# Routing moved into the last dense expert, with a scratch region for every routed expert

## What is computed

```python
x = attention(r, k, v, w, u)                  # [1536 tokens, 384]
P = sinkhorn(exp(x @ w_gate))                 # dense mixture: every token, every expert
x = sum(P[:, e:e+1] * (relu(x @ w1[e]) @ w2[e]) for e in range(8))
xn = x / (norm(x) + 1e-6)                     # routed mixture
logits = xn @ en.T / tau                      # en: 8 unit vectors
idx = argmax(logits, axis=1)
gate = softmax(logits)[token, idx]
out[token] = gate * (relu(x @ w1b[idx]) @ w2b[idx])
```

## Time and profile before

| | us |
|---|---|
| median of 3 runs | 1227.06 (1222.53 to 1227.62) |
| the profiled execution | 1222.38 |
| its span, first to last instruction | 1220.6 |
| PE busy | 1152.3 (94%) |
| DVE busy | 506.7 (42%) |
| ACT busy | 424.8 (35%) |
| POOL busy | 228.2 (19%) |

### The profile page before, as it was taken

One profiled execution on the slowest core, in us unless ns is written; L12 is line 12 of the kernel. 1 busy time (PEld: TensorE's weight loads), 2 busy tenths in 40 slices (PEclk: granted clock), 3 DMA queues, 4 the chain that ended last, 5 costly groups with the idle time before them and its releaser, 6 DMA issues. The chain is left out here.

```text
span 1220.6 us, 18206 instructions
## 1 busy us (share of the span) xinstructions
PE 1152.3 (94%) x6862; PEld 1024.9 (84%) x6862; DVE 506.7 (42%) x881; ACT 424.8 (35%) x860; POOL 228.2 (19%) x229
## 2 busy tenths in 40 slices
PE   6998899999999999999999999999999953999997
PEld 5887769899999998999999899999999822899997
DVE  6777555221222222222212222222222253999996
ACT  4655342212212211211221221222111133988884
POOL 4555252102202201210220220121000013010001
PEclk9889899999999999999999999999999975999999
DMA  9620060200020030020002002000000017999991
GB/s 227 124 59 15 2 204 25 102 2 1 1 104 1 1 104 2 1 104 1 1 16 88 2 1 104 1 1 1 1 1 1 1 65 288 368 374 361 368 354 63
DMA packets 97285, 107.91 MB, mean 88 GB/s; under 512 B 53033, under 2 KB 85710, under 8 KB 97216
## 3 DMA queue, kind: packets, MB, share of 16 engines
q1 hardware_dynamic: 95232, 102.15, 25.3%
q0 software_dynamic: 1984, 4.75, 1.0%
HBM read 98.37 MB, written 9.89 MB: 89 GB/s over the span
## 5 line engine op out<-in xcount | busy, mean ns | idle before, releaser
L809 DVE SCALAR_TENSOR_TENSOR h_lo<-hid,h_hi 128x512 fp32r<-128x512 f32 x192 | 132.8, 691 | 571.9 <-ACT h_hi L745 571.9
L745 ACT ACTIVATE h_hi<-hid 128x512 fp32r<-128x512 f32 x192 | 115.0, 599 | 633.9 <-PE hid L859 633.9
L872 PE MATMUL acc<-w_hi,h_hi 128*128 128x384 f32 x768 | 260.4, 339 | 0.0
L872 PE MATMUL acc<-w_hi,h_lo 128*128 128x384 f32 x768 | 260.1, 339 | 0.0
L872 PE MATMUL acc<-w_lo,h_hi 128*128 128x384 f32 x768 | 259.4, 338 | 0.0
L859 PE MATMUL hid<-x_hi,w_lo 128*128 128x512 f32 x576 | 227.6, 395 | 0.0
L859 PE MATMUL hid<-x_lo,w_hi 128*128 128x512 f32 x576 | 227.3, 395 | 0.0
L859 PE MATMUL hid<-x_hi,w_hi 128*128 128x512 f32 x576 | 226.7, 394 | 0.4 <-issue 0.4
L721 POOL TENSOR_TENSOR w_lo<-raw,w_hi 128x384 fp32r<-128x384 f32 x112 | 114.8, 1026 | 556.1 <-ACT w_hi L737 556.1
L872 PEld LDWEIGHTS acc<-w_lo,h_hi 128*128 128x128 f32 x768 | 144.1, 188 | 8.9
L872 PEld LDWEIGHTS acc<-w_hi,h_hi 128*128 128x128 f32 x768 | 144.1, 188 | 8.1
(11 more groups left out here) (214 smaller groups left out, 1282.1 us busy)
## 6 DMA issues: line engine op xcount, KB each, us to landing
raw<-in_moe_w SPq DMA_DIRECT2D x54, 1536.0 KB, 8.9
rows<-filler SPq DMA_DIRECT2D x19, 194.0 KB, 9.1
m_x<-rows SPq DMA_DIRECT2D x19, 194.0 KB, 5.0
spread_w<-in_w SPq DMA_DIRECT2D x16, 144.0 KB, 3.2
spread_r<-in_r SPq DMA_DIRECT2D x16, 144.0 KB, 2.9
spread_k<-in_k SPq DMA_DIRECT2D x16, 144.0 KB, 3.0
v_sb<-in_v SPq DMA_DIRECT2D x16, 144.0 KB, 3.4
out_y<-m_y,m_token POOLq DMA_INDIRECT x19, 6.9
```

The source lines that it names most:

```text
L745: act.activation(h_hi[st % HB][:, :], hid[st % HB][:, :], ACT.Relu).then_inc(s_hhi, 1)
L809: dve.scalar_tensor_tensor(h_lo[st % HB][:, :], hid[st % HB][:, :], 0.0, h_hi[st % HB][:, :].bitcast(F32), ALU.max, ALU.subtract).then_inc ...
L872: mm = pe.matmul(acc[j][:, 0:DM], a[st % HB][:, j * P:(j + 1) * P], b[q][1][:, f * DM:(f + 1) * DM], start=(f == 0 and x == 0), stop=(f == ...
```

## The change

`route` is gone and its work is spread over the last dense expert (`last_expert` on ACT, DVE and PE).

- **Units.** The 12 tiles form six units (`UNITS`): tiles 0 to 3, tiles 4 to 7, and tiles 8, 9, 10 and 11 by themselves. For each unit run `square` and `roots` on ACT, `turn_tile` on PE, `columns` on ACT, `score` on PE (tiles as the stationary operand, so that logits come out by token), `scales` and `choose` on DVE, `exps` on ACT, `rank` on PE, `weigh` and `locate` on DVE, and one indirect DMA for each tile. Logits are no longer scaled before the maximum; 1/tau is in the expert vectors and the norm in the exponential's scale.
- **Place.** Unit 0 is worked off in steps 9 to 15, unit 1 in steps 17 to 23 and right after. The last group's `hidden` steps run one after the other without `outward` between them, with five more h_hi and h_lo buffers in the space of `x_hi` and `x_lo`; then each of the last four tiles gets its 24 `outward` matmuls in one piece, with the routing of the tile before in between. `keep_clock` puts matmuls whose result nobody reads between the last small ones.
- **Ranks.** A running count `seen` is multiplied in on PE, so a token's row is known when its tile is, because each expert now has a region of 1536 rows in `rows`. The block counts are needed only for slots 8 to 18: slots 0 to 7 are the first block of each expert, in order.
- **Scratch.** `rows` has 12416 rows in place of 2432, filled by one DMA of 2.4 MB for each expert.
- **Weights.** Experts 0 and 1 of the routed mixture are loaded during the last dense expert, and expert 0 is split there by ACT and POOL. In the routed stage slot `s` takes its raw weights from the other buffer, and the splitting of slot 0 is gone.
- **Hand-over.** The wait for the scatters is now SP's, in the routed stage. PE starts that stage with 8 matmuls of 256 fp32 columns (`WARM`) ahead of `turn_x(0)`.

```diff
+        def fill(sp, e):
+            one = slice(e * REGION, (e + 1) * REGION) if isinstance(e, int) else bass.ds(e * REGION, REGION)
+            sp.dma_start(rows[one, :].rearrange("(t p) c -> p t c", p=P),
+                         filler[:, :].unsqueeze(1).broadcast_to([P, REGION // P, ROW])).then_inc(s_fill, 16)
...
-            for n in range(SLOTS):
-                sp.dma_start(rows[n * P:(n + 1) * P, :], filler[:, :]).then_inc(s_fill, 16)
-            sp.wait_ge(s_fill, 16 * SLOTS)
+            sp.dma_start(tau_col[:, :], tau.unsqueeze(0).broadcast_to([E, 1])).then_inc(s_tau, 16)
+            sp.dma_start(rows[E * REGION:E * REGION + P, :], filler[:, :]).then_inc(s_fill, 16)
+            for n in range(2):
+                fill(sp, n)
             with sp.Fori(2, E) as e:
                 sp.wait_ge(s_wlo, (e - 1) * NP)
                 load_expert(sp, w1, w2, e, raw, s_raw)
+                fill(sp, e)
+            sp.wait_ge(s_wlo, LAST * NP)
+            load_expert(sp, w1_next, w2_next, 0, raw, s_raw)
+            sp.wait_ge(s_wlo, E * NP)
+            load_expert(sp, w1_next, w2_next, 1, raw, s_raw2[0])
...
                 split(i * 2 + 2, 0)
             split(E - 1, 1)
+            split(E, 0)
+            pool.wait_ge(s_fill, 16 * (E + 1))
+            for u, (a, b) in enumerate(UNITS):
+                pool.wait_ge(s_gate, u + 1)
+                pool.wait_ge(s_pos, u + 1)
+                for t in range(a, b):
+                    pool.indirect_dma_start(
+                        out=rows, out_offset=bass.IndirectOffsetOnAxis(ap=pos_i[:, t:t + 1], axis=0),
+                        in_=out[:, t, :], in_offset=None).then_inc(s_scat, 16)
...
+            def square(t):
+                act.wait_ge(s_out, LAST * AC + t + 1)
+                if t:
+                    act.wait_ge(s_ssq, t)
+                act.activation(t_sq[:, :], out[:, t, 0:DM], ACT.Square, accum_out=ssq[:, t:t + 1]).then_inc(s_ssq, 1)
+            def roots(u):
+                a, b = UNITS[u]
+                act.wait_ge(s_ssq, b)
+                act.activation(root[:, a:b], ssq[:, a:b], ACT.Sqrt).then_inc(s_root, 1)
+            def columns(t):
+                act.wait_ge(s_tr, t + 1)
+                act.activation(x_cols[t % 2][:, :], bank_of(t)[:, XT:XT + DM], ACT.Copy).then_inc(s_xt, 1)
+            def exps(u):
+                act.wait_ge(s_sh, u + 1)
+                for t in range(*UNITS[u]):
+                    ex = act.activation(expd[:, t, :], shifted[:, t, :], ACT.Exp, scale=scale[:, t:t + 1],
+                                        accum_out=esum[:, t:t + 1])
+                ex.then_inc(s_exp2, 1)
...
+            def last_expert(e, q):
...
+                for t in range(2 * GT, TT):
+                    u = unit_of(t)
+                    square(t)
+                    roots(u)
+                    columns(t)
+                    exps(u)
...
+            def scales(u):
+                a, b = UNITS[u]
+                dve.wait_ge(s_root, u + 1)
+                done[0] = newton(dve, s_rstep, done[0], root[:, a:b], ssq[:, a:b], guess[:, a:b], quot[:, a:b])
+                rstep(dve.reciprocal(scale[:, a:b], quot[:, a:b]))
+            def choose(u):
...
+                dve.wait_ge(s_lg, b)
+                rstep(dve.tensor_reduce(top[:, a:b], lg, AX.X, ALU.max))
+                dve.tensor_tensor(shifted[:, a:b, :], lg, top[:, a:b].unsqueeze(2).broadcast_to([P, n, E]), ALU.subtract).then_inc(s_sh, 1)
+                dve.wait_ge(s_sh, u + 1)
+                flat = hit[:, a:b, :].rearrange("p t e -> p (t e)")
+                rstep(dve.tensor_scalar(flat, shifted[:, a:b, :].rearrange("p t e -> p (t e)"), 0.0, None, ALU.is_ge))
+                rstep(dve.tensor_tensor_scan(order[:, 0:n * E], again[:, 0:n * E], flat, 0.0, ALU.mult, ALU.add))
+                dve.scalar_tensor_tensor(flat, order[:, 0:n * E], 1.0, flat, ALU.is_equal, ALU.mult).then_inc(s_hit, 1)
+            def weigh(u):
+                a, b = UNITS[u]
+                dve.wait_ge(s_exp2, u + 1)
+                rstep(dve.tensor_scalar(esum[:, a:b], esum[:, a:b], 1e-9, None, ALU.add))
+                dve.reciprocal(out[:, a:b, DM], esum[:, a:b]).then_inc(s_gate, 1)
+            def locate(u):
...
+            def last_expert(e):
...
+                        locate(0)
+                scales(1)
+                choose(1)
+                weigh(1)
+                locate(1)
+                tail_add(2 * GT)
+                for t in range(2 * GT, TT):
+                    u = unit_of(t)
+                    scales(u)
+                    choose(u)
+                    if t + 1 < TT:
+                        tail_add(t + 1)
+                    weigh(u)
+                    locate(u)
...
-            with dve.Fori(1, E) as e:
...
+            def turn_tile(t):
+                pe.wait_ge(s_out, LAST * AC + t + 1)
...
+                for k in range(KD):
+                    mm = pe.transpose(bank_of(t)[:, XT + k * P:XT + (k + 1) * P], out[:, t, k * P:(k + 1) * P], ident[:, :])
+                mm.then_inc(s_tr, 1)
+            def score(t):
...
+                pe.wait_ge(s_xt, t + 1)
+                for k in range(KD):
+                    mm = pe.matmul(bank_of(t)[:, at:at + E], x_cols[t % 2][:, k * P:(k + 1) * P], e_cols[:, k, :],
+                                   start=(k == 0), stop=(k == KD - 1), skip_group_check=True)
+                mm.then_inc(s_lg, 1)
+            def rank(u):
...
+                bank = bank_of(a)
+                pe.wait_ge(s_hit, u + 1)
+                if u:
+                    pe.wait_ge(s_seen, u)
+                tokens = lambda c: hit[:, a:a + c, :].rearrange("p t e -> p (t e)")
+                mm = pe.matmul(bank[:, RK:RK + n * E], upper[:, :], tokens(n), start=True, stop=False, skip_group_check=True)
+                for d in range(1, n):
+                    mm = pe.matmul(bank[:, RK + d * E:RK + n * E], ones[:, :], tokens(n - d), start=False, stop=False,
+                                   skip_group_check=True)
+                for d in range(n):
+                    mm = pe.matmul(bank[:, RK + d * E:RK + (d + 1) * E], ones[:, :], seen[u][:, :], start=False, stop=True,
+                                   skip_group_check=True)
+                mm.then_inc(s_rank, 1)
+            def last_expert(e, q):
...
+                for st in range(TAIL, FL - 1):
+                    hidden(e, q, st + 1)
+                    if TAIL + 2 <= st < TAIL + 2 + GT:
+                        score(st - TAIL - 2 + GT)
+                    if TAIL + 1 <= st < TAIL + 1 + GT:
+                        turn_tile(st - TAIL - 1 + GT)
+                for j in range(GT):
+                    t = TAIL // KF * GT + j
+                    pe.wait_ge(s_out, e * AC + (NG - 2) * GT + j + 1)
+                    for f in range(KF):
+                        st = TAIL + f
+                        if j == 0:
+                            pe.wait_ge(s_hlo, e * FL + st + 1)
+                        for x, (a, b) in enumerate(((h_hi, hi), (h_hi, lo), (h_lo, hi))):
+                            h = h_buf(a, x_hi if a is h_hi else x_lo, st)
+                            mm = pe.matmul(acc[j][:, 0:DM], h[:, j * P:(j + 1) * P], b[q][1][:, f * DM:(f + 1) * DM],
+                                           start=(f == 0 and x == 0), stop=(f == KF - 1 and x == 2))
+                        if f == KF - 1:
+                            mm.then_inc(s_tacc, 1)
+                        if f == 1:
+                            if j == 0:
+                                rank(1)
+                            if j >= 2:
+                                rank(unit_of(t - 2))
+                            if j >= 1:
+                                turn_tile(t - 1)
+                        if f == 5 and j >= 1:
+                            score(t - 1)
+                keep_clock(2)
+                rank(unit_of(TT - 2))
+                turn_tile(TT - 1)
+                keep_clock(2)
+                score(TT - 1)
+                keep_clock(3)
+                rank(unit_of(TT - 1))
+                pe.wait_ge(s_seen, len(UNITS))
+                pe.matmul(logits[:, RK + E:RK + 2 * E], ones[:, :], seen[len(UNITS)][:, :], start=True, stop=True,
+                          skip_group_check=True).then_inc(s_tot, 1)
+            def keep_clock(n):
+                pe.wait_ge(s_out, LAST * AC + 2 * GT + 1)
+                for _ in range(n):
+                    pe.matmul(acc[0][:, 0:256], ident[:, :], filler[:, 0:256], start=True, stop=True, skip_group_check=True)
...
-def route(nc, w1, w2, e_cols, tau, out, rows, ident, ones, upper, slot_expert, experts_known, raw, hi, lo, s_raw, s_hi1, s_w1):
...
                 if there(s):
-                    if there(s - 1):
-                        e = expert_of(s)
-                    one = slice(s * P, (s + 1) * P) if isinstance(s, int) else bass.ds(s * P, P)
```

(34 more changed lines are left out.)

423 lines of the change are left out of this document (198 added, 225 removed).

## The result

The changed kernel took **1214.86 us** (median of 7 runs, 1211.52 to 1219.98); the kernel before, on the same chip, 1224.97 us (7 runs, 1222.23 to 1227.62). The ratio is 0.9926, 95% interval 0.990 to 0.9952: faster by 0.7%, some 9 us; the two medians lie 10.1 apart. The forecast was 1213.4, as 13.7 us less than 1227.06. The time misses it by only 1.5 us and the gain by 3.6, because the kernel before has the lower median here: that closeness is luck. The profiled execution took 1214.86 us, span 1212.4.

The account below looks back on a forecast made before the run. PE was taken as busy except around 995 to 1032 us, the only place to gain. Slot 1 at 1020.5 against 1036.9 gave 16.4 us; less 2.7 for one clock drop, 13.7 gained: 1213.4 us, range 1207 to 1224.

Parts of the forecast that it names:

- rival A: Whole kernel: the forecast, one clock drop in the tail; 1213.4 us, own range 1209 to 1218; chance 0.47.
- Part 1, S: Last dense expert: S, the last hidden's relu, stays near 971.2; -12.6 outward moved, +7.1 small products, +5.2 score waits.
- Part 2: First of the last four tiles: PE waits 2.8 us at rank(1); a clock drop from it costs 2.7 us.
- Part 3: Three more tiles: PE sets the pace at 5.2 us each, covering ACT's 4.4 us including table loads.
- Part 4: End of last tile: table done 33.0 us, last scatter landed 34.0 us after the last dense hidden's relu.
- Part 5: Routed stage start: WARM takes 6.7 us, ending 3.4 us after slot 0's rows arrive; slot 0's products take 4.2 us.
- B: Tail: no clock drop, or a short WARM; 16 to 19 us gained, 1208 to 1211 us; chance 0.20.
- C: Tail: three to five clock drops from the score waits, 2.7 us each; 1219 to 1224 us; chance 0.15.
- D: Last tiles: an equally long pause follows each table load, ACT 7.0 us a tile; 1222 us; chance 0.05.
- E: Clock falls at the first score wait, stays at 1.2 GHz to WARM's end; about 1247 us; chance 0.05.
- F: Routed slots get longer, 0.9 us each, as DVE and DMA lack reserve; 1229 us; chance 0.08.
- At no cost: Fills growing from 3.7 to 21.5 MB, expert 0's splitting and SP's extra register read cost no time.

Follow-up runs that it names:

- E0: Not a run but an event: the last dense expert's first relu; at 875.02 and 872.76 us in two executions of the kernel before.
- e1: Changed kernel with ACT's columns, square and root of unit 1 one step earlier; median 1212.53 us, ratio 0.9898 to the kernel before.
- e2: Changed kernel with DVE's scales and choice of unit 1 after step 22, not 23; median 1209.54 us, ratio 0.9895 to the kernel before.
- e8: Changed kernel with the edits of e1, e2 and e5 together; median 1202.14 us, ratio 0.9833 to the kernel before.
- e11: e8 with slot 1's w1 split before slot 0's row is there; median 1201.84 us, ratio 0.9824 to the kernel before.
- e10: Changed kernel with the edits of e1 and e2, without the bridge of e5; one time, 1207.1 us.
- e6: Changed kernel with a copy in place of the exponential in tiles 8 to 11 (gates wrong); one time, 1213.05 us.
- e4: Changed kernel with the table for slots 8 to 18 counted in the routed stage; median 1214.79 us, ratio 0.9933 to the kernel before.
- the twelve kernels: The changed kernel and its eleven edited variants, each profiled; no single time.
- e9: Changed kernel with slot 1's weights fetched in the routed stage, as in the kernel before; one time, 1219.84 us.
- e5: Changed kernel with eight more keep-clock products bridging the change of stage and WARM 8 to 5; median 1215.94 us, ratio 0.9946 to the kernel before.

## Why the prediction was right, and where it was off

The forecast was rival A, and A is what happened, with the five parts 0.4 to 2.4 us off. Predicted distance 148.2 (161.9 - 13.7), measured 152.9:

- **Part 1, S.** Predicted all but unchanged (-0.3), measured +2.1 (S - E0 from 96.51 to 98.58). The waits were priced at 5.2; without them S comes 5.3 earlier (e1), so that price held, though a gap shows only 1.07 of its 1.33. The small products were underpriced: by subtraction 2.1 + 12.6 - 5.3 = 9.4, not 7.1. A tile's transposes and scores take 0.93 behind a `hidden` without a wait (3.03 - 2.1 in e1), not 0.75, and eight ranks 1.8 (974.84 to 976.65 in e2, at full clock), not 1.1. The failed price is the product with 8 columns: I took 0.14 for both passes from a 96-column row, where it is about 0.2; the upper bound of 0.28 was there. The mechanism, a wait per score with the next `hidden` queued behind it, held (e1).
- **Part 2 and the clock drop.** The wait was priced at 2.8 and is 2.61. First tile, with the one drop of 2.7: S + 10.8, measured S + 11.9. The drop came where I put it. In e2, e8 and e11, with waits of 0.33 and 0.18, there was none; in e10, with 0.18, the clock fell all the same. So the long wait was followed by a drop each time it was there, but it is not shown to be the only cause.
- **Part 3.** PE sets the pace, as said, at 5.3, 5.6 and 5.6 in place of 5.2 (+0.9), again the small products. e6 confirms that the table loads of tiles 8 to 10 are covered.
- **Part 4.** From the last add to SP's load 11.0 us, predicted 10.3. The table on DVE is not on the path to SP's load, as said (e4). But I let the change of stage follow the table, at S + 33.0, and so put `WARM` 0.8 ahead of SP's load. It does not: `WARM` starts 0.05 after SP's load, and both come 0.8 to 0.9 us behind the landing of POOL's last scatter (e4).
- **Part 5.** From SP's load to slot 1's first product 14.9, predicted 15.3. `WARM` ended 6.0 after the load, against 5.9 as worked out, and that is luck: it started 0.8 later than I had it and took 5.96, not 6.7.
- Sum of the misses: +2.4, +1.1, +0.9, +0.7, -0.4 = 4.7. In whole times the gain is 10.1 by the medians, 3.6 short, and some 9 by the ratio.

The rivals: B (no drop) did not occur, though e8 shows that it is to be had. C: two drops, ahead of 986 and at 1014, and both were in the sum; the score waits drew none (1.00 from 900 to 976). D: tiles would be 7 us apart and are 5.3 to 5.6, and the gaps around a load are 0.02 and 0.01. The Trainium skill ("ScalarE: Activation LUTs", "What ACT_TABLE_LOAD costs") states a drain of some 1.38 us with each load; the trace does not agree. E: no long stretch at 1.2 GHz. F: the slots kept 9.56 us (1038.74 to 1048.30), and DVE and DMA even have a little less to do (155.54, 0.90).

"At no cost" holds for the fills. They write 19.3 MB (eight of 2.38 MB and one of 0.2), not 21.5 as I had it, and from the first dense relu to E0 it is 706.2 to 707.3 us in the twelve kernels, 706.9 and 706.5 in the two profiles of before. What I had left out is that the early fetch of slot 1's weights would bring nothing beside a long `WARM` (e9). The time from slot 0's first product to slot 1's fell from 10.3 and 8.9 in the two executions of before to 7.3. Against the second all of it is the clock of slot 0's products, 5.9 and 4.3; the 3.0 behind them are the same. Against the first, some 0.5 is the wait for the weights.

One cost I had not thought of lies in the attention stage, whose code is the same. There the twelve kernels differ from the two profiles of before in one direction: the loads of 144 KB land after 3.6 to 4.3 us (medians), not 2.9 to 3.4, for the same packets and bytes; PE's first product comes at 6.5 to 6.8, not 6.1; the first dense product at 164.4 to 171.9, not 162.5 and 164.5. Windows of before, then of the changed kernel:

```profile
0.00:40.00 40.00, 28.55 (x336) 23.84 (x336) 24.81 (x48) 21.98 (x65) 22.04 (x31) 0.99 0.89 210
120.00:168.00 48.00, 40.38 (x385) 31.23 (x385) 25.45 (x44) 20.83 (x59) 20.34 (x17) 0.86 0.06 17
```
```profile
0.00:40.00 40.00, 26.96 (x270) 21.99 (x270) 23.09 (x42) 19.57 (x55) 20.22 (x29) 0.91 1.12 201
120.00:168.00 48.00, 41.74 (x457) 32.37 (x458) 26.79 (x49) 23.22 (x70) 21.28 (x19) 0.83 0.03 5
```

The DMA engines have the larger share for fewer GB/s. So the later E0 (878.3 on average over twelve, 873.9 over two) arises ahead of the dense experts. It is probably a small cost of the change: of the eight kernels with several times, seven gain less in the whole time than in the distance, by 0.4 to 3.3 us. No run tried what makes the loads slower.

What stays open: why the clock fell in e10 and not in e8; why the rows land after 2.4 to 4.5 us; and why the attention stage's loads are slower.

## What to carry to other kernels

Work moved under a busy engine is worth its distance in the queue: what hurt here were five places where PE met an operand whose producer had started too late. They were mended by moving the producer and not PE's work: 8.8 us for both moves together (e10), 14.3 with the bridge, in an execution in which the clock held and the rows came early (e8). A wait of 2.6 us on PE has to be priced twice, as the wait and as the slow products that came behind it each time. Fillers that keep the clock pay only when they end after the data arrive: with the same bridge the turn waited 2.1 us in e5, and 1.1 was lost; in e8 it did not wait, and 3.6 was won; in e11 the data were 0.5 late, and slot 0's products took 1.5 more. And a distance between two events is read by its parts: two executions agreed to 0.15 us while their parts moved by 1.4.
